# Chunk 1's first unit finished ahead of the first copies, GpSimd's second weights released by it, softmax groups in steps 12 to 17

## What is computed

```python
w = exp(weight_gen - max(weight_gen)); w = w / (sum(w) + 1e-9)   # over the 7 taps
a[b, s] = sum over k of w[b, s, :, k] * x_pad[b, s + k, :]       # per head, group of 24
h = a @ w_in          # 8192 x 192 @ 192 x 2048
y = (h * cos(h)) @ w_out
h = y @ w2_in
out = max(0.01 * h, h) @ w2_out
```

## Time and profile before

| | before |
|---|---|
| median of 3 runs | 1149.82 us |
| lowest, highest | 1148.96, 1151.4 us |
| profiled execution, own time | 1150.26 us |
| its span in the trace | 1148.5 us |
| mean granted TensorE clock | 0.998 |
| TensorE matmul busy | 1130.3 us (98%) |
| VectorE busy | 934.7 us (81%) |
| ScalarE busy | 726.1 us (63%) |
| GpSimd busy | 87.2 us (8%) |

### The profile page before, as it was taken

How to read it: one execution, slowest core, us unless ns; L and a number is a source line. 1 busy time by engine, 2 the same in 40 slices (tenths; PEclk the granted TensorE clock), 3 DMA queues, 4 the chain that set the end, 5 groups by cost and what they waited for, 6 DMA issues and landing times.

```text
span 1148.5 us, 22931 instructions
## 1 busy us (share of the span) xinstructions
PE 1130.3 (98%) x9766; PEld 943.0 (82%) x9766; DVE 934.7 (81%) x911; ACT 726.1 (63%) x774; POOL 87.2 (8%) x80
## 2 busy tenths in 40 slices
PE   7899999999999999999999999999999999999998
PEld 5777888888888888888888888888888888888876
DVE  8999798888979889797896969879797896978443
ACT  6666675766657666575755747566575655757553
POOL 5860000000000000000000000000000000000000
PEclk9999999999999999999999999999999999999999
DMA  9660201103011020301102011020201103010001
GB/s 261 199 130 1 63 2 35 43 1 77 1 39 39 12 66 1 77 1 33 45 1 77 1 38 40 12 65 1 51 27 31 47 1 77 1 38 6 1 15 29
DMA packets 85118, 48.41 MB, mean 42 GB/s; under 512 B 58140, under 2 KB 78490, under 8 KB 84632
## 3 DMA queue, kind: packets, MB, share of 16 engines
q1 hardware_dynamic: 80568, 41.70, 14.1%
q0 software_dynamic: 4448, 5.24, 2.6%
HBM read 35.12 MB, written 11.80 MB: 41 GB/s over the span
## 4 chain that ended last, share of the span: by engine, by line
PE 90%; DVE 3%; ACT 1%; issue 1%; ACTq 0%; DVEq 0%
PE slot L1186 42%; PE acc_a L1186 28%; PE acc_b L1186 19%; DVE g_lo L909 1%; DVE prods L317 0%; DVE prods L326 0%; ACT g_hi L717 0%; PE acc_b L1159 0%; ACT gate L787 0%; ACT L847 0%; DVE gate L1007 0%; PE acc_a L1152 0%; PE acc_b L1160 0%; PE acc_a L1151 0%; ACT taps_w L847 0%
## 5 line engine op out<-in xcount | busy, mean ns | idle before, releaser
L1186 PE MATMUL acc_a<-g_hi,out_hi_lo 64*128 64x512 f32 x2000 | 697.2, 388 | 0.0
L909 DVE TENSOR_TENSOR g_lo<-gate,g_hi 128x1024 fp32r<-128x1024 f32 x252 | 310.0, 1231 | 118.3 <-ACT g_hi L717 118.0
L1186 PEld LDWEIGHTS acc_a<-g_hi,out_hi_lo 64*128 64x128 f32 x2000 | 368.6, 184 | 35.3
L1186 PE MATMUL acc_b<-g_hi,out_hi_lo 64*128 64x512 f32 x1000 | 388.7, 389 | 6.7 <-DVE g_lo L909 3.1
L1186 PE MATMUL acc_a<-g_lo,out_hi_lo 64*128 64x512 f32 x1000 | 387.0, 387 | 0.0
L1186 PE MATMUL acc_b<-g_lo,out_hi_lo 64*128 64x512 f32 x1000 | 386.8, 387 | 0.0
L717 ACT ACTIVATE g_hi<-gate 128x1024 fp32r<-128x1024 f32 x252 | 267.7, 1062 | 98.8 <-PE acc_b L1186 76.4
L1186 PE MATMUL slot<-x_a_hi,in_a_lo 64*128 64x512 f32 x1024 | 297.6, 389 | 1.0 <-DVE g_lo L909 0.7
L1186 PE MATMUL slot<-x_b,in_b_hi 64*128 64x512 f32 x1024 | 296.5, 387 | 0.2 <-DVE x_b L931 0.2
L1186 PE MATMUL slot<-x_a_lo,in_a_hi 64*128 64x512 f32 x1024 | 296.4, 387 | 0.1
L1186 PE MATMUL slot<-x_a_hi,in_a_hi 64*128 64x512 f32 x1024 | 296.5, 387 | 0.0
(11 more groups left out here) (109 smaller groups left out, 1022.3 us busy)
## 6 DMA issues: line engine op xcount, KB each, us to landing
x_win<-in_x SPq DMA_DIRECT2D x14, 960.0 KB, 4.9
x_columns<-prods SPq DMA_DIRECT2D x56, 96.0 KB, 2.0
out<-turned_a SPq DMA_DIRECT2D x240, 16.0 KB, 1.5
x_raw_a<-x_columns SPq DMA_DIRECT2D x14, 256.0 KB, 2.9
out<-turned_b SPq DMA_DIRECT2D x120, 16.0 KB, 1.5
result<-x_columns SPq DMA_DIRECT2D x14, 128.0 KB, 3.0
out_raw<-in_moe_w_out SPq DMA_DIRECT2D x3, 512.0 KB, 8.4
out_hi_lo<-in_moe_w_out POOLq DMA_DIRECT2D x2, 768.0 KB, 11.4
```

The lines of the kernel that those rows point to most:

```text
L909: nc.vector.tensor_tensor(g_lo[:, q % 2, :], result_of(i - b, q), g_hi[:, q % 2, :].bitcast(FP32), ALU.subtract)\
L1186: return nc.tensor.matmul(to, w[rows, :], x[rows, :], start=start, stop=stop)
```

## The change

It has three parts. First, in step (1, 0) VectorE does the four last softmax parts of group 2 (so far at (0, 9)), then the product of unit (1, 0) ahead of folding acc_b, and g_lo of that unit at the end of the same step; ScalarE makes g_hi of that unit ahead of copying acc_a. Second, GpSimd's low parts of layer two's weights wait for that g_lo in place of the softmax part. Third, the groups 3 to 5 of the softmax lie wholly in iterations 1, 3 and 5: max at step 12, subtract at 13, exp at 14, sum at 15 with the sine's table, guard and invert at 16, multiply at 17. So far they were max and subtract at (1, 8), or at steps 13 and 14 of iterations 2 and 4, exp at 10, the table at 12, sum at 13, guard and invert at 14, multiply at 16.

```diff
-        EXP_STEP, SINE_STEP = 10, 12
+        EXP_STEP, SINE_STEP = 14, 15
...
-        SOFT_AT = {(0, 9): [(2, part) for part in TAIL_PARTS]}
-        for n, (begin, end) in enumerate(((1, 1), (2, 3), (4, 5)), 2):
-            SOFT_AT[begin, 8 if n == 2 else 13] = [(n, "max")]
-            SOFT_AT.setdefault((begin, 8 if n == 2 else 14), []).append((n, "subtract"))
-            SOFT_AT[end, 13] = [(n + 1, "sum")]
-            SOFT_AT[end, 14] = [(n + 1, "guard"), (n + 1, "invert")]
-            SOFT_AT[end, 16] = [(n + 1, "multiply")]
+        SOFT_AT = {}
+        for n, i in enumerate((1, 3, 5), 2):
+            SOFT_AT[i, 12] = [(n, "max")]
+            SOFT_AT[i, 13] = [(n, "subtract")]
+            SOFT_AT[i, 15] = [(n + 1, "sum")]
+            SOFT_AT[i, 16] = [(n + 1, "guard"), (n + 1, "invert")]
+            SOFT_AT[i, 17] = [(n + 1, "multiply")]
...
-            pool.wait_ge(soft, soft_count(2, "multiply"))
+            pool.wait_ge(lo_ready, unit(1, 0) + 1)
...
             def pending_high(i, step):
                 b, prev = back(step, 1)
-                if is_unit(i - b, prev):
+                if (i, step) != (1, 1) and is_unit(i - b, prev):
                     high_part(i - b, UNITS.index(prev))
...
+                if (i, step) == (1, 0):
+                    high_part(1, 0)
                 j = first_out(i, step)
                 if j is not None:
                     act.wait_ge(summed, unit(j, 7) + 1)
...
+            def product(i, q):
+                slot = slots[UNITS[q] % SLOTS][:, :, :].rearrange("p a n -> p (a n)")
+                dve.wait_ge(cos_ready, first_units(i, q))
+                nc.vector.scalar_tensor_tensor(result_of(i, q), slot, RADIANS, gate[:, q % 2, :],
+                                               ALU.mult, ALU.mult).then_inc(g_ready, 1)
+
+            def low_part(i, q):
+                dve.wait_ge(hi_ready, unit(i, q) + 1)
+                nc.vector.tensor_tensor(g_lo[:, q % 2, :], result_of(i, q),
+                                        g_hi[:, q % 2, :].bitcast(FP32), ALU.subtract)\
+                    .then_inc(lo_ready, 1)
+
             def pending_low(i, step):
                 b, prev = back(step, 1)
-                if is_unit(i - b, prev):
+                if (i, step) != (1, 1) and is_unit(i - b, prev):
...
                 pending_low(i, step)
+                if (i, step) == (1, 0):
+                    for part in TAIL_PARTS:
+                        softmax(2, part)
+                    product(1, 0)
                 j = first_out(i, step)
...
-                elif in_first:
...
+                elif in_first and (i, step) != (1, 0):
+                    product(i, q)
+                if (i, step) == (1, 0):
+                    low_part(1, 0)
                 if i < LAST:
                     split_second_low(i, step)
```

More of the change, by code:

```diff
@@ L907, in pending_low @@
                         return
[L908 to L911, removed]
+                    low_part(i - b, q)
             def split_low(step, chunk):
```

## The result

The changed kernel takes 1157.81 us (median of five runs, 1156.25 to 1159.02), the kernel before 1150.53 (five runs, 1148.96 to 1151.4). The ratio is 1.0062 (95% interval 1.0051 to 1.0072), 7.3 us slower. The profiled execution took 1158.83 us itself, 8.57 more than that of before. It lies at the slow end of its five, and 1.9 us of the 8.57 were lost ahead of anything that the change touches (the fifth pair at 53.68 was at 51.80 in before).

What follows compares the result with a forecast made beforehand. TensorE, 90% of the chain, was taken to bound the kernel. Handover -1.6, max and subtract -0.9, softmax groups +7.0 gave +4.5 on the profiled 1150.26: 1154.8, or 1154.3 in the median; range 1151.2 to 1157.0.

Steps and rivals of the forecast that it cites:

- Part 1: Handover at unit (1,0): 2.1 us of TensorE's stall goes, 0.5 comes at unit (1,1); together -1.6.
- what is late next: After the handover, unit (1,1): its g_lo ends at 76.2, its sum due at 75.93; costs 0.5 with refill.
- Part 2: Max and subtract leave (1,8), shortening the stall at layer two's first sum (mid_b): -0.9 us, bounds 0 and -1.7.
- the sum: All three parts added against the profiled 1150.26: -1.6 - 0.9 + 7.0 = +4.5 us, so 1154.8.
- Part 3: Softmax groups moved to iteration ends delay the next chunk's input split: cost 8.3 us, less 1.3 regained, +7.0.
- The fold of step 1: VectorE's fold after iterations 3 and 5: some 0.8 us late, hidden by the split's wait; without that, costs 1.6.
- The range: Total time from 1151.2 (three stalls of 2, both gains whole) to 1157.0 (late g_lo, stalls of 3.4).
- late g_lo: Rival at unit (1,1): g_lo asks after GpSimd's in_b_lo has begun; total +6.0 us, 1155.8; chance 0.36.
- estimate of 1162.6: Forecast if six table switches also drained about 1380 ns each, by the skill page: 8.3 us more; not adopted.
- split in time: Rival at the next chunk's input split: no delay there; total -2.2 us, 1147.6; chance 0.10.
- half split: Rival at the input split: late by half of what was counted; total +0.4 us, 1150.2, no change; chance 0.12.

Runs made afterwards that it cites:

- e2: Kernel before with only the new places of softmax groups 3 to 5, old handover and GpSimd wait: 1157.17 us, ratio 1.006.
- e1: Changed kernel with softmax groups 3 to 5 back at their old steps; handover and GpSimd's wait stay: 1151.81 us, ratio 1.0007.
- e3: Changed kernel with the sine's table reload at step 16, behind the split, in place of 15: 1157.19 us, ratio 1.0064.
- e5: Changed kernel with 9, 12 and 12 extra matmuls on weights in TensorE's stalls at the split: 1156.46 us, ratio 1.0053.
- e8: The kernel before, unchanged, run once more: 1151.08 us in one run.
- e6: Changed kernel with exp at step 12, sine and sum at 13, guard and invert at 14, multiply at 16, max and subtract earlier: 1147.49 us, ratio 0.9976.
- e4: Changed kernel with exp at step 13, sine at 16, sum at 14, guard and invert at 15, multiply at 16: 1152.14 us, ratio 1.0009.
- e7: e6 with GpSimd's last six of eight output weight pieces waiting for layer one's last g_lo: 1149.75 us, ratio 0.9993.
- e10: e6 with GpSimd's wait before layer two's weights put back to the softmax part: 1147.24 us, ratio 0.9965.

## Why the prediction was wrong in size

**The handover (Part 1, -1.6): -0.8 measured, and nothing once mid_b is counted.** The gain of 2.1 and the 0.5 at (1,1) came as worked out, and the order of g_lo and in_b_lo by a lead of 0.1 to 0.2 us too. The step that failed is "what is late next": I looked for it at (1,1) alone. The 1.8 us of VectorE's waits for GpSimd over units 1 to 5 stood in Part 2 as a price for mid_b only; in between they also brought g_lo of (1,4) 0.7 late. And the two parts share one gain: together they are -1.67 in after (-2.5 in the sum), and e2 has -1.74 without the handover.

**Max and subtract (Part 2, -0.9): -0.85.** Right, and e1, which leaves them at (1,8), has mid_b at 2.53 over the period, 1.65 more than after: the 1.66 that the two take. That the rest of the stall stays only because TensorE comes earlier is borne out by e2, where it doesn't come earlier and the whole 1.73 goes.

**The softmax groups (Part 3, +7.0): +6.5 without the clock** (2.0 + 6.0 - 1.5). Term by term it was right to 0.3 us, and e2 confirms that the loss is this part's. One reason given was too narrow: I let ScalarE alone set the split, with VectorE's sum adding 0.2. e3 shows VectorE's chain to be 0.3 us shorter and no more. The fold of step 1 stays hidden as foreseen: at 429.04 it still waits 0.92 us for TensorE.

**The term that was missing: the clock behind a stall**, 1.63 in this profile and some 2.0 in the median by e5 beside after, which is an estimate. This is the step that failed most: the prediction put the term at nothing. It took a stall's price to be its length and 0.1 for refilling, as the stall of 1.8 at 73.59 shows it, whose period is 6.43. One place in one execution was too little for that. e8 has the same stall with 1.6 us more in its period, and the trace of before itself held the other case, at the very first sum, which I had not read: TensorE there, and the window around it.

```profile
32.13 0.72 PE L1186 MATMUL acc_b<-g_hi,out_hi_lo 64*128 64x512 f32 x1 [2.23 <-DVE g_lo L904]
```

```profile
32.00:34.00 2.00, 1.87 (x10) 1.76 (x12) 2.00 (x3) 0.81 (x1) 2.00 (x2) 0.54 0.76 303
```

For the profiled execution, counted from the fifth pair of fill (1,3), the account closes by measured terms: the prediction's 4.5, with 0.7 for (1,4), 1.63 for the clock, and less 0.37 for what the other terms were off, gives 6.46 of the 6.61. The 7.3 of the medians is 0.7 more. The estimate of 2.0 for the clock would fill half of that, but it was itself worked out from the 7.3 and confirms nothing; what the start of the program adds to the median no run shows.

**The range.** Its ends don't follow one rule. Stalls of 2 at three places with both gains whole are 6.0 - 1.3 - 2.1 - 1.7 = +0.9: 1151.2 against the profiled 1150.26, but 1150.7 in the median. Late g_lo and three stalls of 3.4 are 10.2 - 1.3 + 0.7 - 1.7 = +7.9, in the median 1157.7; 1157.0 holds only with 2.7 for the first of the three. Neither end had room for the clock.

**The rivals.** The late g_lo did not occur. The split in time and the half split did not either. e6, whose groups lie elsewhere, has its split in time and at 1147.5 lies by luck where that rival's arithmetic put it (1147.6): the rival counted +1.6 for the fold, which costs nothing in e6, and -1.6 for the handover, where e6 has -0.9. Table loads without a drain: 408.20 plus 1.28 is 409.48 and the exponential starts at 409.50, as the earlier trace rows had it, so no drain shows beside the load, and the estimate of 1162.6, by the section "What ACT_TABLE_LOAD costs" of the Trainium skill's "ScalarE: Activation LUTs", fell.

**Open.** No run shows why the clock fell behind the 3.0 of iteration 5 in after, e2 and e3, and not behind the equal one of iteration 3 in after, and behind the 1.8 in e8 but not in before. In the eight profiles whose stalls were left empty (before, after, e1 to e4, e7, e8), 16 periods behind fill (1,3) lose 1.8 us or more, and the clock fell behind 4 of them. Nothing that these runs show tells the 4 from the 12. The start is open too: in after's profile the clock was at 0.50 from 24 to 26 us, in that of before at 0.54 from 32 to 34, and over all the other profiles the fifth pair of fill (1,3) lies between 70.99 and 72.67. The clock alone does not decide it: it fell near the start in before, after, e3, e4 and e6 (71.39, 73.27, 72.48, 71.98, 71.78) and not in the others (70.99 to 72.67). What decides it within one execution no run shows.

## What to carry to other kernels

Put a table switch and its exponential where the ScalarE queue waits for another engine anyway (here behind g_hi of step 12), and trace both engines' queues up to the next deadline: when the first chain is cleared the second may be as long. Price a stall of 2 to 3 us of a steadily busy TensorE at its length plus up to 1.6 us (here behind one such stall in four), and read several executions before taking that term for nothing. A stall removed early on is only a gain if the engines behind it can follow; here the handover alone gave its 2.1 us back within 40 us, and two gains that end in the same wait are one gain.

## What the runs showed of the hardware

- Behind stalls of 1.8 to 3.3 us the granted clock fell to 0.50 for some 3.4 us in 4 cases of 16, in after while TensorE was busy for 2.00 of 2.00 us in both slow windows (matmuls 0.62 for 0.39 us). That cost 1.3 (e2) to 1.65 us (e3) where nothing absorbed it. Matmuls issued into the stalls kept it at 1.000 in five runs of five (e5).
- A VectorE instruction that waits for GpSimd gets in when GpSimd's instruction ends, though GpSimd's next one is already queued: in_b_lo took 3.38 us in place of 2.38 with g_lo of (1,1) ahead of it, and in e10 g_lo of (1,0) took 1.21 between two pieces of in_a_lo, the second of which took 3.51 for 2.40. In after g_lo at 80.49 waited for a GpSimd piece of 0.73 that had begun at 80.46 and took 1.78 for 1.23, and the next piece took 2.27 for 1.30. The Trainium skill, "SBUF — State Buffer", section "Who interferes with whom", has one of the two block the other for a whole instruction; the rows agree. In these traces a VectorE instruction so lost at most 1.25 us at one meeting (g_lo in before, 2.48 for 1.23), and which of the two engines stood hung on which came first, by 0.18 us at in_b_lo.
